# GpSimd subtracts the softmax maximum, a new order on all engines, and x stored in pieces between the W loads

## The reference, cut to what matters

```python
def attention(q, k, v, phi):              # q, k, v (8, 8, 576, 64); phi (8, 8, 576, 32)
    a = phi - max(phi, axis=2); a = exp(a); a = a / (sum(a, axis=2) + 1e-9)
    k_m = einsum('bhsm,bhsd->bhmd', a, k);  v_m = einsum('bhsm,bhsd->bhmd', a, v)
    scores = matmul(q, k_m.T) / 8
    scores = scores - max(scores, -1);  attn = exp(scores)
    attn = attn / (sum(attn, -1) + 1e-9)
    return matmul(attn, v_m)
def moe1(x, w_in, w_out):                 # x (4608, 512), w_in (512, 2048), w_out (2048, 512)
    h = x @ w_in
    return (h * sigmoid(1.702 * h)) @ w_out
def moe2(x, w_gate, w_output_gate, w1, w2):
    # 8 experts (512 x 1024 and 1024 x 512), one for each token
```

## Time and profile before

| | us |
|---|---|
| median of 3 runs | 1333.48 (1333.1 to 1334.02) |
| the profiled execution | 1334.72 |
| its span, first to last instruction | 1333.0 |
| PE busy, share of the span | 1309.6, 98% |
| DVE busy | 629.7, 47% |
| POOL busy | 548.4, 41% |
| ACT busy | 388.3, 29% |
| mean granted clock of TensorE | 0.995 of 2.4 GHz |

### The profile page before, as it was taken

The page is one execution under the profiler, slowest core; times in us unless marked ns, Lnnn a source line. Parts: engine busy times, 40 slices in busy tenths (PEclk is TensorE's granted clock), DMA queues, the critical chain, the costliest instruction groups (busy, mean ns, idle before and its releaser), DMA issues.

```text
span 1333.0 us, 23549 instructions
## 1 busy us (share of the span) xinstructions
PE 1309.6 (98%) x6872; PEld 1053.5 (79%) x6873; DVE 629.7 (47%) x1291; ACT 388.3 (29%) x725; POOL 548.4 (41%) x649
## 2 busy tenths in 40 slices
PE   7999999999999999999999999999999999999998
PEld 3447888888888888888888888887788888888886
DVE  5893343434433434334434344347555555555553
ACT  4663232222222322222222222223322222222221
POOL 2567944444433434334334343412443242433332
PEclk8999999999999999999999999999999999999999
DMA  9997456575465554654655646647873789549882
GB/s 380 416 405 278 127 201 192 194 194 199 159 180 194 166 178 169 189 174 172 179 185 174 180 170 184 199 159 232 256 206 101 221 238 258 166 128 257 249 247 71
DMA packets 153418, 274.18 MB, mean 206 GB/s; under 512 B 17363, under 2 KB 54612, under 8 KB 150804
## 3 DMA queue, kind: packets, MB, share of 16 engines
q1 hardware_dynamic: 96676, 203.21, 45.2%
q10 hardware_dynamic: 43728, 38.55, 11.8%
q0 software_dynamic: 12960, 31.72, 7.7%
HBM read 144.92 MB, written 100.45 MB: 184 GB/s over the span
## 4 chain that ended last, share of the span: by engine, by line
PE 92%; DVE 3%; DMA 2%; issue 1%; ACT 1%; ACTq 0%; POOL 0%; SPq 0%; POOLq 0%
PE ps L717 29%; PE ps L750 29%; PE ps L820 16%; PE ps L791 15%; DMA phT<-in_phi 2%; PE ps L760 1%; PE ps L628 1%; DVE sc L1173 1%; DVE scs L1175 1%; DVE scs L1184 0%; PE ps L681 0%; ACTq L1046 0%; PE ps L653 0%; DVE sc L1177 0%; DMA cq<-ch 0%
## 5 line engine op out<-in xcount | busy, mean ns | idle before, releaser
L717 PE MATMUL ps<-xs,W 128*128 (+1 forms) x1728 | 417.5, 390 | 0.0
L750 PE MATMUL ps<-W,gs 128*128 128x512 f32 x1728 | 415.0, 389 | 0.1
L717 PEld LDWEIGHTS ps<-xs,W 128*128 128x128 f32 x1728 | 322.9, 188 | 69.7 <-issue 3.1
L750 PEld LDWEIGHTS ps<-W,gs 128*128 128x128 f32 x1728 | 324.2, 188 | 67.8 <-DVE gs L1239 0.5
L1237 DVE TENSOR_TENSOR gate<-ps,gate 128x512 f32<-128x512 f32 x144 | 99.5, 691 | 369.9 <-ACT gate L988 369.9
L988 ACT ACTIVATE gate<-ps 128x512 f32<-128x512 f32 x144 | 86.1, 598 | 467.8 <-PE ps L717 467.3
L820 PE MATMUL ps<-W,chT 128*128 (+1 forms) x936 | 218.3, 389 | 1.5 <-DVE chT L1374 1.5
L791 PE MATMUL ps<-W,cx 128*128 (+1 forms) x936 | 218.5, 389 | 0.4 <-issue 0.4
L1617 POOL CAST whi<-raw 128x512 fp32r<-128x512 f32 x128 | 83.1, 649 | 328.2 <-DMA raw<-in_moe_w 328.2
L820 PEld LDWEIGHTS ps<-W,chT 128*128 128x128 f32 x936 | 175.6, 188 | 38.8 <-issue 2.3
L791 PEld LDWEIGHTS ps<-W,cx 128*128 128x128 f32 x936 | 175.5, 188 | 37.3 <-issue 1.0
(11 more groups left out here) (159 smaller groups left out, 779.9 us busy)
## 6 DMA issues: line engine op xcount, KB each, us to landing
W<-expert_scratch SPq DMA_DIRECT2D x24, 2048.0 KB, 11.2
raw<-in_moe_w SPq DMA_DIRECT2D x128, 256.0 KB, 2.8
expert_scratch<-whi SPq DMA_DIRECT2D x128, 256.0 KB, 2.7
expert_scratch<-raw SPq DMA_DIRECT2D x128, 256.0 KB, 3.0
cq<-ch ACTq DMA_DIRECT2D x156, 128.0 KB, 3.8
kvm<-in_kv SPq DMA_DIRECT2D x15, 1152.0 KB, 9.9
crec<-record_scratch POOLq DMA_DIRECT2D x160, 64.0 KB, 3.4
qT<-in_q SPq DMA_DIRECT2D x16, 576.0 KB, 8.2
```

Source lines behind the costliest of these rows:

```text
L717: mm = pe.matmul(ps[:, f % 2, :], W[:, col:col + P], xs[:, bass.ds(x0 + (x_lo * K1 + c) * T, T)], start=(c == 0 and w_lo + x_lo == 0), sto ...
L750: mm = pe.matmul(ps[:, 2 + s, :], gs[:, f % 2, g_lo, s * P:(s + 1) * P], w_out_sb[:, f, w_lo, :], start=(f == 0 and g_lo + w_lo == 0), sto ...
```

## The change

DVE's subtraction of the scores' maximum goes to GpSimd for all groups but the last. phi is loaded and reduced two groups ahead in place of one. The exps of phi and scores, the copies and the transposes change places on ACT, DVE and PE; k and v are summed in PSUM bank 0 in place of bank 4. Three warm-up matmuls stand where one stood. hi of x's first two pieces goes to GpSimd. At the end of attention one more `mm1` and one more w_out split come early, and the first sigmoid stands ahead of the last exp of the scores. The W chunks come in order of use, two or more w_out chunks, then four pieces of w_in; x is stored by half batches between them, the first store with half the bytes. The wait for all stores of x leaves DVE, and on ACT moves to the end of the first tile.

```diff
+        def n_out(f):
+            return K1 + 8 * (f // 4) + (0, 1, 6, 7)[f % 4] if f < 12 else 16 + f
+        def n_in(c, k):
+            return K1 + 8 * (k - 1) + 2 + c if k else c
+        def first_half_stored(eng):
+            eng.wait_ge(s_xu0, 16 * (KEPT - FIRST + 1))
+            eng.wait_ge(s_x10, 16)
         def kept_stored(eng):
-            eng.wait_ge(s_xfirst, 16 * 2)
-            eng.wait_ge(s_xkept, 16 * 2 * (KEPT - FIRST))
+            first_half_stored(eng)
+            eng.wait_ge(s_x11, 16)
+            eng.wait_ge(s_xu1, 16 * (KEPT - 2))
...
# SP
+            load_phi(1)
             load_q(0)
+            load_phi(2)
             for g in range(1, NG):
-                load_phi(g)
                 load_kv(g)
                 load_q(g)
+                if g + 2 < NG:
+                    load_phi(g + 2)
...
-            for c in range(2):
-                load_w(K1 + 2 * c, w_out_v[c])
-                load_w(K1 + 2 * c + 1, w_in_part(c, 1))
-            store_kept(0, FIRST, s_xfirst)
+            load_w_out(0)
+            load_w_out(1)
+            load_w_in(0, 1)
+            load_w_in(1, 1)
+            store_kept(0, FIRST, 0, s_xu0)
...
+                    load_w_in(2, 1)
+                    store_kept(FIRST, 1, 0, s_xu0)
+                    load_w_in(3, 1)
+                    store_kept(FIRST + 1, 1, 0, s_xu0)
+                    load_w_out(2)
+                    store_kept(0, 1, 1, s_x10)
+                    load_w_out(3)
+                    store_kept(1, 1, 1, s_x11)
+                    load_w_out(4)
...
+                    sp.wait_ge(s_o, 2 * NG)
+                    load_x(t + 1)
+                    load_w_out(5)
+                    store_kept(2, 1, 1, s_xu1)
+                    for c in range(K1):
+                        load_w_in(c, 2)
+                        store_kept(3 + c, 1, 1, s_xu1)
...
# PE
             def group(g):
+                kv_product(g)
+                if g >= 3:
+                    out_half(g - 3, 0)
+                k_transposes(g)
+                if g + 1 < NG:
+                    a_main(g + 1)
+                    pe.wait_ge(s_kmT, g + 1)
+                    a_rest(g + 1)
+                scores(g)
                 if g >= 3:
                     out_half(g - 3, 1)
...
-            a_transposes(0)
-            warm_up(1)
-            for g in range(NG):
+            a_main(0)
+            a_rest(0)
+            warm_up(3)
+            kv_product(0)
+            k_transposes(0)
+            scores(0)
+            a_main(1)
+            a_rest(1)
+            for g in range(1, NG):
                 group(g)
...
             mm1(0, 0)
             out_half(NG - 3, 1)
+            mm1(0, 1)
             out_half(NG - 2, 0)
-            mm1(0, 1)
             out_half(NG - 2, 1)
+            mm1(0, 2)
             for i in range(2):
                 out_half(NG - 1, i, (6, 4)[i])
-            mm1(0, 2)
+            mm1(0, 3)
...
# ACT
             def group(g):
                 u = g % 2
-                if g + 1 < NG:
-                    exp_phi(g + 1, 1 - u)
+                kv_scale(g, u)
                 if g >= 4:
                     x_out(g - 4, 1)
-                if g >= NG - 2:
-                    for c in range(2):
-                        first_x_hi(2 * (g - (NG - 2)) + c)
-                kv_scale(g, u)
+                k_out(g)
+                if g == 0:
+                    exp_phi(1)
+                if g >= 3:
+                    x_out(g - 3, 0)
+                if g + 1 < NG:
+                    a_out(g + 1)
                 if g:
                     exp_scores(g - 1, 1 - u)
-                k_out(g)
-                if g + 1 < NG:
-                    a_out(g + 1)
-                if g >= 3:
-                    x_out(g - 3, 0)
+                if g + 2 < NG:
+                    exp_phi(g + 2)
+                if g == NG - 2:
+                    first_x_hi(2)
+                    first_x_hi(3)
...
-            exp_scores(NG - 1, 1)
-            x_out(NG - 3, 1)
-            x_out(NG - 2, 0)
-            g_step(0, 0)
-            x_out(NG - 2, 1)
+            g_sigmoid(0, 0)
+            exp_scores(NG - 1, 1)
+            x_out(NG - 3, 1)
+            g_hi(0, 0)
+            g_sigmoid(0, 1)
+            for i in range(2):
+                x_out(NG - 2, i)
+            g_hi(0, 1)
...
# DVE
             def group(g):
-                u = g % 2
-                if g + 1 < NG:
-                    phi_in(g + 1)
-                inverses(g, u, g >= 2, True)
-                if g:
-                    less_max(g - 1, 1 - u)
+                scores_in(g - 1, (g - 1) % 2)
+                inverses(g - 2 if g >= 2 else None, g + 1 if g + 1 < NG else None)
+                scores_max(g - 1, (g - 1) % 2)
+                if g + 2 < NG:
+                    phi_in(g + 2)
                 if g >= 2:
                     attn_out(g - 2)
...
# GpSimd
             for g in range(NG):
+                if g - 1 in QUARTER:
+                    c = QUARTER.index(g - 1)
+                    split_w_in(c, c, 0)
+                if g >= NG - 2:
+                    x_first(g - (NG - 2))
                 if g >= 2:
                     normalize(g - 2, g % 2)
+                if g:
+                    less_max(g - 1, 1 - g % 2)
                 v_blocks(g, g % 4)
-                if g in QUARTER:
-                    c = QUARTER.index(g)
-                    split_w_in(c, c, 0)
-                if g == NG - 2:
-                    for c in range(2):
-                        first_x_lo(c)
-            first_x_lo(2)
-            normalize(NG - 2, 0)
+            pool.wait_ge(b_xhi, 1)
+            x_first_lo(2)
             pool.wait_ge(s_x3, 1)
             pool.wait_ge(b_xlo, K1 - 1)
+            pool.sem_inc(b_xhi, 2)
             pool.sem_inc(b_xlo, 1)
+            split_w(n_out(0), 0)
+            normalize(NG - 2, 0)
```

More of the change, by code:

```diff
@@ L521, in sp_tile @@
                 if first:
[L522 to L542, removed]
@@ L543, in sp_tile @@
-                    for f in range(12, C1):
-                        load_w(16 + f, w_out_v[f])
+                    load_w_in(2, 1)
[7 more added lines that the diff above has]
+                    load_w_out(4)
+                    sp.wait_ge(s_xu0, 16)
@@ new lines, in sp_tile @@
+                    sp.dma_start(stage[0], cst["before"]).then_inc(s_cst2, 16)
+                    sp.dma_start(stage[1], gates).then_inc(s_cst2, 16)
+                    sp.wait_ge(b_setup, 1)
+                    sp.dma_start(padrec[:].bitcast(I32)[:, DM + NE + 1:DM + NE + 2], cst["padtoken"]).then_inc(b_cst, 16)
+                    load_w_out(8)
+                    load_w_out(9)
+                    for c in range(K1):
+                        load_w_in(c, 3)
+                    for f in range(10, C1):
+                        load_w_out(f)
@@ L825, in pe_tile @@
                 for f in range(STEPS):
-                    if not first or f >= 3:
+                    if not first or f >= 4:
                         mm1(t, f)
-                    if f:
+                    if first and f == 4:
+                        mm2(t, f - 2)
+                    if f and not (first and f == 3):
                         mm2(t, f - 1)
-                    elif not first:
+                    if f == 0 and not first:
                         mm2(t - 1, C1 - 1)
@@ L915, in kv_scale @@
                 wait(act, s_vbd, g)
-                act.activation(kvs[:], ps[:, 4, 3 * P:4 * P], ACT.Copy, scale=scs[:, u, 2, SB:SB + 1]).then_inc(s_kk, 1)
+                act.activation(kvs[:], ps[:, 0, 3 * P:4 * P], ACT.Copy, scale=scs[:, 1 - u, 2, SB:SB + 1]).then_inc(s_kk, 1)
             def k_out(g):
@@ L1073, in act_tile @@
                         load_x(t + 1)
-                    if not first or f:
+                    if not first or f >= 2:
                         g_step(t, f)
                     if first and f == 2:
-                        stage_a_done(act)
+                        act.wait_ge(s_xst, 16)
+                    if first and f == STEPS - 1:
+                        kept_stored(act)
                     if not first:
@@ L1088, in act_tile @@
                         x_hi(t + 1, f - 11)
-            g_step(0, 0)
-            x_out(NG - 2, 1)
-            x_out(NG - 1, 0, 6)
-            x_out(NG - 1, 1, 4)
+            g_sigmoid(0, 0)
[6 more added lines that the diff above has]
+            g_hi(0, 1)
+            for i in range(2):
+                x_out(NG - 1, i, (6, 4)[i])
             store_last()
@@ L1240, in g_step @@
                                   ALU.subtract).then_inc(b_glo, 1)
+            scores_in(NG - 1, 1)
+            dve.wait_ge(b_xhi, 2)
+            dve.tensor_tensor(xs[:, (2 * K1 - 1) * T:2 * K1 * T], kept(K1 - 1), xs[:, (K1 - 1) * T:K1 * T].bitcast(F32),
+                              ALU.subtract).then_inc(s_x3, 1)
+            inverses(NG - 2)
+            scores_max(NG - 1, 1)
```

(18 more changed lines are left out.)

155 lines of the change are left out of this document (95 added, 60 removed).

## The result

The changed kernel takes 1331.01 us (median of 18 runs, 1329.42 to 1333.0); the kernel before, in the same job, 1333.51 (18 runs, 1332.13 to 1335.18). The ratio is **0.9981, 95% interval 0.9975 to 0.9987**: faster by 2.5 us. The profiled execution took 1330.6 us, with a span of 1329.0 at a mean granted clock of 1.000.

What follows compares the result with a forecast made beforehand. DMA was taken to bound attention, DVE and TensorE within 5%, and TensorE the dense part. First mm2 3.4 us earlier took the profiled 1334.72 to 1331.3; the median's 1.24 made it 1330.1, range 1326.9 to 1334.2.

Steps and rivals of the forecast that it cites:

- Subtraction on GpSimd: Attention: fifteen of sixteen subtractions leave DVE, 11.6 us less, at 1.16 us each on GpSimd; 1.5 to 2 us for the stage.
- The ring: Attention, each plain group: exps, DVE's small steps, normalization and subtraction follow each other in a cycle of 4.63 us, against 4.90.
- Order at the start: Start of attention: a blocked phi load leaves the DMA queues dry from 18.4 to 19.9; +1.5 us on all later loads.
- End of attention: The last group's product: 88.6 by data, 88.8 by the engines, taken as 89.5 us against 90.76 before.
- K: The instant at which attention ends, with the last group's product; forecast 89.5 us.
- The tail: From K to the first mm2: 17.9 us of TensorE's path, plus 0.5 and 0.6, 19.0; mm2 at 108.5, gain 3.4.
- W chunks and x in pieces: First tile: GpSimd's 2.1 us per W chunk and the split stores of x stay hidden; cost nothing.
- the 111.9 of the kernel before: First mm2 of the kernel before, 109.20 with three mm1 done, set at 111.9 with a fourth; compared with 108.5.
- Given back: Rival, 28%: attention ends earlier, but PE idles between groups and gets the half clock again; gain 1.7, 1331.8 us.
- The data's pace alone: Rival, 15%: attention follows its loads, nothing slips, no dry queues; first mm2 at 105.5, gain 6.4, 1327.1 us.
- the 1.24 us: Whole kernel: the shown median, 1333.48, lay 1.24 us below the profiled execution, taking 1331.3 to 1330.1.
- GpSimd the bound: Rival, 12%: GpSimd's stretched operations make an attention group 5.4 us; first mm2 at 116.3, 4.4 late, 1337.9 us.

Runs made afterwards that it cites:

- experiment 10: The changed kernel with a second operation of the same form, subtracting zeros, ahead of each GpSimd subtraction in groups 0 to 14; 1345.88 us.
- experiment 3: The changed kernel with the subtraction of groups 0 to 14 back on DVE behind the maximum, every other order kept; 1335.41 us.
- experiments 1 and 2: 1: the changed kernel with phi's second exp ahead of group 0 on ACT, 1329.37 us. 2: the changed kernel with one warm-up instead of three, 1329.56 us.
- experiment 5: The changed kernel with the last exp ahead of the first sigmoid on ACT, and group 15's inverses ahead of the sigmoid product on DVE; 1329.62 us.
- experiment 6: The changed kernel with x of the first five batches stored at once in both halves instead of in pieces; 1331.58 us.
- experiment 11: The changed kernel again, unchanged; 1330.59 us.
- experiment 7: The changed kernel with one warm-up instead of three and normalization 14 ahead of the W split on GpSimd; 1329.40 us.
- experiment 8: The kernel before, unchanged, profiled a second time; 1333.24 us.
- experiments 7 and 9: 9: the kernel of experiment 7 with the first store of x waiting on SP until product 15 is done; 1328.66 us. 7 has its own line.
- experiment 4: The kernel before, in its old order, with the subtraction of groups 0 to 14 on GpSimd behind the normalization; 1332.77 us.

## Why the prediction was right, and what in it was not

The forecast was 1330.1, with 1326.9 to 1334.2; 1331.01 was measured, faster by 0.19%. That is 2.50 us, just under the 2.67 that I had called the least a measurement can tell; 18 runs of each kernel tell it. By its own steps:

1. *Subtraction on GpSimd.* Right in price (1.159 for 1.16) and in relief (DVE 4.10 for 4.2). The ring was 4.42, not 4.63. That a ring, not the sum of GpSimd's work, sets the limit is shown by experiment 10. The Trainium skill's rule ("GPSIMD Engine Reference", section 4.1) that speaks against the move has a ratio of about 2; the rows have 1.16 against 0.77, 1.5, and experiment 3 shows the reverse of the rule in this place: with the subtraction on VectorE the kernel is 4.4 us slower (1335.41 against 1331.01; 0.36% by the ratios), because VectorE had nothing to spare and GpSimd had.
2. *Order at the start.* Right in place and size. phi 4 was issued at 18.05 (forecast 18.7), the dip lay at 18 to 19, kv 14 landed 1.9 and kv 15 2.8 us later than before, and experiments 1 and 2 give back 1.2 to 1.5.
3. *End of attention.* K = 89.8, forecast 89.5, but by another way: the data came in at 88.3 rather than 87.05, and the product followed 1.5 later. That it is so near is luck: in experiments 5, 6 and 11 K is 88.7 to 89.1, by data in at 86.8 to 87.1, and the product follows 1.9 to 2.0 later.
4. *The tail.* First mm2 at 108.1 for 108.5, 18.3 us after the product for 19.0; but in experiments 5, 6 and 11 it is 19.1 to 19.4 after it, and the instant is the same. The size is right and the path is not: I hung the tail on K, and what comes last starts at kv 14 and runs through group 15's softmax on DVE and GpSimd. What lengthens it has a place, the W split ahead of normalization 14 and the stretched operations behind it: without them (experiment 7) TensorE works through in 18.0, my bare 17.9. The table loads are hidden (experiment 5).
5. *W chunks and x in pieces.* Nothing, as said (experiment 6).

The mis-sized term is the other side of the subtraction: **the 111.9 of the kernel before**. I took its first mm2, 109.20, from one execution that lost 1.6 us to a half clock near it, and so made the gain 3.4; with 110.3 from experiment 8 it is 2.2, and 2.5 was measured. Then I took the 1.24 us by which that execution stood above its median off once more. These are one thing counted twice: what the disturbed execution had lost, the change can't win.

The rivals. *Given back* priced a half clock in the changed kernel that didn't come, and table loads in the open; both are refuted here by the profiles, and only by them: its 1331.8 is 0.8 from the result, the forecast 0.9. *The data's pace alone* would need the dry spell gone and a shorter tail: experiments 7 and 9 come nearest, 106.3 and 106.1 for its 105.5. *GpSimd the bound* is a real mechanism, seen in experiment 10, 0.5 us a group away.

What stays open: how much of experiment 4's lateness is the order of ACT and how much the half clock in the middle of its one profile; and how much of the gain of the change is that the clock no longer falls in attention.

## What to carry to other kernels

An engine's idle share is not its room: find the ring that it stands in, add up one turn, and compare it with the period of whatever binds; here 1.7 us of idle time a group were 0.5 us of room. In a queue that issues in order, look at what the first blocked issue waits for, because a spell of empty queues early in a stage that is bound by its data comes out at its end (here kv 14 landed 1.9 us later). And before a gain is read off one profile, look at the granted clock near the instant that counts, or take the instant from a second execution; and when two paths end within a fraction of a microsecond, one execution's chain doesn't tell which of them sets the time.

## What the runs showed of the hardware that I had not expected

- Two-input operations on DVE and GpSimd stretch each other: DVE's subtraction 0.757 alone and 1.21 beside the normalization (experiment 3), the normalization 1.69 for 1.16 in the tail. The Trainium skill ("GPSIMD Engine Reference", "1. Specifications") says that GpSimd shares its SBUF interfaces with VectorE and contends with VectorE's instructions that have two SBUF inputs; the rows agree, and give the size, 1.5 to 1.6 times.
- The granted clock of TensorE differs between executions of one kernel. In attention it falls at different instants (42 to 46 and 93 to 97 in the first profile of before, 30.4 to 33.8 in the second, 42 to 49 in experiment 4), and only for the stretch at 93 is a cost at the end shown.
- Most of what scatters between executions of this kernel lies in a part that the change doesn't touch. From the first mm2 to the end of the span it is 1220.9 us in the changed kernel's first profile and 1223.8 in experiment 5's. The 55 us from the last sigmoid of MoE 1, in the first and then in the other, and in each the matmuls in their middle:

```profile
887.00:942.00 55.00, 52.64 (x265) 42.40 (x264) 36.57 (x122) 19.63 (x39) 16.73 (x25) 1.00 0.74 240
919.76 11.21 PE L878 MATMUL ps<-W,chT 128*128 128x512 f32 x48 [1.08 <-DVE chT L1469]
```
```profile
886.90:941.90 55.00, 50.72 (x252) 41.06 (x252) 35.82 (x119) 18.89 (x36) 14.88 (x21) 0.97 0.73 231
921.98 12.55 PE L878 MATMUL ps<-W,chT 128*128 128x512 f32 x48 [3.38 <-DVE chT L1469]
```

  TensorE waits 2.3 us longer for DVE there, and then the clock is granted at 0.5 from 921 to 925. Two more profiles have both the wait (2.00 us in experiment 11, 3.28 in experiment 3) and the half clock behind it, and need 1222.5 and 1225.1 us to the end; the other six of the new order (experiment 10 aside) need 1220.8 to 1221.7. So the instant of the first mm2 is the sharper measure of such a change than one execution's time.
